# Recurrent attention with two mixtures of experts: the first expert's G spread in block order, with both spreadings ahead of the copies

## What is computed

```python
B, H, S, D = 4, 8, 768, 48            # attention; tokens = B*S = 3072, width = H*D = 384
for t in range(S):                    # state: (B, H, D, D)
    cur = einsum('bhd,bhe->bhde', u * k[t], v[t])
    y[t] = einsum('bhd,bhde->bhe', r[t], state + cur)
    state = w * state + einsum('bhd,bhe->bhde', k[t], v[t])
x = y as (3072, 384)
logits = x @ phi                      # 32 slots: 8 experts x 4
d, c = softmax(logits, 0), softmax(logits, 1)
slot_out[e] = relu((d.T @ x)[e] @ w1[e]) @ w2[e]
x = c @ slot_out                      # (3072, 384), rank 32
logits = x @ w_gate                   # 8 experts, top 1
e = argmax(logits, 1); g = softmax(logits, 1)[e]
out[n] = g[n] * (relu(x[n] @ w1b[e]) @ w2b[e])      # F = 1024 inner columns
```

## Time and profile before

| | |
|---|---|
| median of 3 runs | 275.95 us (275.84 to 276.87) |
| the profiled execution's own time | 276.53 us |
| its span, first to last instruction | 274.8 us |
| mean granted clock of TensorE, as a share of full | 0.975 |
| busy: PE, DVE, ACT, POOL | 95%, 56%, 32%, 11% |
| HBM traffic over the span | 200 GB/s |

### The profile page before, as it was taken

The page is one execution under the profiler, slowest core; times in us unless marked ns, Lnnn a source line. Parts: engine busy times, 40 slices in busy tenths (PEclk is TensorE's granted clock), DMA queues, the critical chain, the costliest instruction groups (busy, mean ns, idle before and its releaser), DMA issues.

```text
span 274.8 us, 10456 instructions
## 1 busy us (share of the span) xinstructions
PE 262.1 (95%) x4509; PEld 220.7 (80%) x4509; DVE 155.0 (56%) x322; ACT 89.3 (32%) x175; POOL 30.6 (11%) x45
## 2 busy tenths in 40 slices
PE   7979899999999998999999799999999999999996
PEld 6767687888787884433469599999999999999995
DVE  7957788888988874435030585353533522525323
ACT  1224445545545543031230453222222222222200
POOL 3312122222222215000000000000000000000000
PEclk9979999999999999999995979999999999999999
DMA  5955899999999999999507500030030200300303
GB/s 158 374 178 196 281 324 377 398 384 397 396 401 397 327 417 416 425 371 425 249 2 262 198 2 0 0 116 0 0 114 0 80 35 0 114 0 0 117 0 120
DMA packets 16260, 55.30 MB, mean 201 GB/s; under 512 B 1872, under 2 KB 5136, under 8 KB 15344
## 3 DMA queue, kind: packets, MB, share of 16 engines
q1 hardware_dynamic: 13152, 43.90, 42.7%
q10 hardware_dynamic: 3088, 11.14, 10.6%
HBM read 50.31 MB, written 4.72 MB: 200 GB/s over the span
## 4 chain that ended last, share of the span: by engine, by line
PE 91%; DVE 4%; issue 2%; ACT 1%; POOL 0%; DVEq 0%; POOLq 0%
PE ps L1207 12%; PE ps L1208 12%; PE ps L1206 12%; PE ps L939 8%; PE ps L962 6%; PE ps L977 6%; PE ps L986 5%; PE ps L951 5%; PE ps L1191 4%; PE ps L1077 4%; PE ps L1099 4%; PE ps L991 3%; PE ps L896 3%; PE ps L1046 2%; PE ps L1108 1%
## 5 line engine op out<-in xcount | busy, mean ns | idle before, releaser
L829 DVE SCALAR_TENSOR_TENSOR hl<-ps,hh 128x512 fp32r<-128x512 f32 x48 | 32.9, 690 | 58.5 <-ACT hh L571 58.5
L1207 PE MATMUL ps<-w2l,hh 128*128 128x384 f32 x192 | 65.2, 340 | 0.0
L1208 PE MATMUL ps<-w2h,hl 128*128 128x384 f32 x192 | 65.0, 338 | 0.0
L1206 PE MATMUL ps<-w2h,hh 128*128 128x384 f32 x192 | 64.9, 338 | 0.0
L571 ACT ACTIVATE hh<-ps 128x512 fp32r<-128x512 f32 x48 | 28.6, 598 | 75.6 <-PE ps L1191 75.6
L1207 PEld LDWEIGHTS ps<-w2l,hh 128*128 128x128 f32 x192 | 36.4, 190 | 1.6
L1206 PEld LDWEIGHTS ps<-w2h,hh 128*128 128x128 f32 x192 | 36.5, 190 | 0.7
L1208 PEld LDWEIGHTS ps<-w2h,hl 128*128 128x128 f32 x192 | 36.5, 190 | 0.0
L438 POOL TENSOR_TENSOR kt<-intk,kttab 128x384 f32<-128x384 f32 x24 | 24.2, 1008 | 71.1 <-DVE rkb L643 52.2
L643 DVE TENSOR_TENSOR rkb<-ind,tab 128x1024 f32<-128x1024 f32 x24 | 29.8, 1242 | 0.2 <-DMA ind<-dmaj 0.2
L939 PE MATMUL ps<-rkb 64*64 64x128 f32 x768 | 28.2, 279 | 0.0
(11 more groups left out here) (167 smaller groups left out, 304.0 us busy)
## 6 DMA issues: line engine op xcount, KB each, us to landing
ind<-dmaj SPq DMA_DIRECT2D x22, 512.0 KB, 7.8
wearly<-wa ACTq DMA_DIRECT2D x21, 512.0 KB, 7.2
intk<-tmaj SPq DMA_DIRECT2D x24, 384.0 KB, 6.8
wearly<-wa SPq DMA_DIRECT2D x4, 1536.0 KB, 10.4
out<-acc SPq DMA_DIRECT2D x5, 768.0 KB, 3.6
wlate<-wa SPq DMA_DIRECT2D x4, 768.0 KB, 8.8
wlate<-wa SPq DMA_DIRECT2D x2, 1536.0 KB, 11.3
wmid<-wa SPq DMA_DIRECT2D x1, 1536.0 KB, 8.6
```

Of the source, the lines that this page charges most:

```text
L829: v.scalar_tensor_tensor(out=hl[:, f % 4, :], in0=ps[:, f % 4, :], scalar=0.0, in1=hh[:, f % 4, :].bitcast(F32), op0=ALU.max, op1=ALU.subt ...
L1206: mm(o, a_h, w2h[:, f, :], start=(f == 0), stop=False)
L1207: mm(o, a_h, w2l[:, f, :], start=False, stop=False)
L1208: ins = mm(o, a_l, w2h[:, f, :], start=False, stop=(f == KF - 1))
```

## The change

Four things are edited. (1) G's columns: strip j now takes blocks j and j+4 (`w1cols`, a view of the same weights with two runs of 128 columns), so spreading 0 yields blocks 0 to 3 and spreading 1 blocks 4 to 7; `gstv` follows. (2) Both spreadings are issued back to back, then all copies: every copy of ScalarE waits for the third `gg_done` and every copy of VectorE for the fourth, so each of these engines copies both halves in a row. The first four `h1` are in block order; the first waits for ScalarE's first copy, the second for VectorE's first, the fourth for both second copies. (3) ScalarE makes `w2_high(0)` ahead of its copies instead of behind the first. (4) Products of ones: 3 new ones ahead of the wait for the last part of `cs`, 16 in place of 8 among the 24 gate products, none in place of 6 behind the gate, 2 new ones between the three parts of G, 1 new one behind the spreadings and 2 behind the four `h1`. The diff:

```diff
--- before.py
+++ after.py
@@ -157,7 +157,8 @@
                     piece[2 * e + 1].rearrange("p (f d) -> p f d", f=KF))
 
         w1raw = wraw[:, 0, :].rearrange("p (k f) -> p k f", k=KD)
-        gstv = gst[:, :].rearrange("p (j i n) -> p j i n", j=4, i=2)
+        w1cols = wraw[:, 0, :].rearrange("p (k i j n) -> p k j i n", k=KD, i=2, j=4)
+        gstv = gst[:, :].rearrange("p (i j n) -> p j i n", j=4, i=2)
         w2raw = wraw[:, 1, :].rearrange("p (f d) -> p f d", f=KF)
 
 
@@ -548,7 +549,7 @@
 
                 def g_copy(i):
 
-                    sc.wait_ge(gg_done, k * 4 + 2 * i + 1)
+                    sc.wait_ge(gg_done, k * 4 + 2 + 1)
                     a.activation(gstv[:, 0:2, i, :],
                                  ps[:, 4:6, i * P:(i + 1) * P], ACT.Copy).then_inc(gst_ready[2 * i], 1)
 
@@ -557,10 +558,9 @@
                     sc.wait_ge(w2b_in[first // 2], k * 16 + 16)
                     a.activation(w2h[:, first:end, :], w2raw[:, first:end, :], ACT.Copy).then_inc(w2h_done, 1)
 
-                def high(u, f, place=None):
-
+                def high(u, f):
                     n = k * NU + u
-                    sc.wait_ge(h_done, n * KF + (f if place is None else place) + 1)
+                    sc.wait_ge(h_done, n * KF + f + 1)
 
                     if f < 3:
                         sc.wait_ge(l2_done, n * (KF - 1) + f - 2 + L20)
@@ -572,12 +572,12 @@
 
                 sc.wait_ge(g_done, k + 1 + 1)
                 a.activation(gh[:, :], ps[:, 3, 0:F // 4], ACT.Copy).then_inc(gh_ready, 1)
+                w2_high(0)
                 g_copy(0)
-                w2_high(0)
+                g_copy(1)
                 high(0, 0)
-                g_copy(1)
                 w2_high(1)
-                high(0, 1, 2)
+                high(0, 1)
                 for p in range(2, len(W2P)):
                     w2_high(p)
                     high(0, 2 * p - 2)
@@ -813,7 +813,7 @@
 
                 def g_copy(i):
 
-                    dve.wait_ge(gg_done, k * 4 + 2 * i + 2)
+                    dve.wait_ge(gg_done, k * 4 + 4)
                     v.tensor_copy(gstv[:, 2:4, i, :],
                                   ps[:, 6:8, i * P:(i + 1) * P]).then_inc(gst_ready[2 * i + 1], 1)
 
@@ -1142,12 +1142,12 @@
             pe.wait_ge(gws_ready, 1)
             pe.wait_ge(cs_ready, 1)
             mm(ps[:, 4, 0:E], cs[:, 0:P], gw[:, :], start=True, stop=True).then_inc(gate0_done, 1)
+            warm(3, 6)
             pe.wait_ge(cs_ready, 6)
             for q in range(NT):
-                warm(q % 3 // 2, 6)
+                warm((q + 1) % 3 // 2 + q % 3 // 2, 6)
                 ins = mm(ps[:, 5, q * E:(q + 1) * E], cs[:, q * P:(q + 1) * P], gw[:, :], start=True, stop=True)
             ins.then_inc(gate_done, 1)
-            warm(6, 6)
 
 
             def expert(k, first):
@@ -1167,10 +1167,12 @@
                 pe.wait_ge(hl_done, k * J + 1)
                 pe.wait_ge(acc_done, k * NT + ACC0)
                 for q in range(KD):
+                    if first and q:
+                        warm(1, 0)
                     pe.wait_ge(w1b_in[q], k * 16 + 16)
                     for j in range(4):
                         ins = mm(ps[j * NS:(j + 1) * NS, 3, 0:W], sot[:, q, j * NS:(j + 1) * NS],
-                                 w1raw[:, q, j * W:(j + 1) * W], start=(q == 0), stop=(q == KD - 1),
+                                 w1cols[:, q, j, :, :], start=(q == 0), stop=(q == KD - 1),
                                  skip_group_check=True, tile_position=(0, j * NS))
                 ins.then_inc(g_done, 1)
                 if first:
@@ -1181,11 +1183,15 @@
                     warm(1, 0)
 
                 g_spread(0)
+                g_spread(1)
+                if first:
+                    warm(1, 2)
 
                 def h1(u, f, lead=False):
 
                     if lead:
-                        pe.wait_ge(gst_ready[f % 2 * 2], k + 1)
+                        if f < 2:
+                            pe.wait_ge(gst_ready[f], k + 1)
                     else:
                         pe.wait_ge(hl_done, (k * NU + u) * KF + f - 3 + 1)
                     mm(ps[:, f % 4, :], gst[:, f * P:(f + 1) * P],
@@ -1211,13 +1217,13 @@
                     if f < KF - 1:
                         ins.then_inc(l2_done, 1)
 
-                h1(0, 0, True)
-                h1(0, 2, True)
-                pe.wait_ge(gst_ready[1], k + 1)
-                g_spread(1)
-                pe.wait_ge(gst_ready[3], k + 1)
-                h1(0, 1, True)
-                h1(0, 3, True)
+                for f in range(4):
+                    if f == 3:
+                        pe.wait_ge(gst_ready[2], k + 1)
+                        pe.wait_ge(gst_ready[3], k + 1)
+                    h1(0, f, True)
+                if first:
+                    warm(2, 4)
                 with pe.Fori(0, NU - 1) as u:
                     for f in range(KF):
                         h2(u, f)
```

## The result

The changed kernel takes 273.44 us (median of 20 executions, 271.59 to 277.15), the kernel before 276.14 us on the same chip (20 executions, 272.57 to 279.26). The ratio is 0.9935, 95% interval [0.9911, 0.9958]: 1.8 us, 0.65%, less. That ratio leaves out executions more than 1.5% above the fastest of their kernel, eight of the twenty of the kernel before and one of the changed one; by the medians of all 20 and 20 it is 0.990, 2.7 us less. Either way it is faster, and by clearly less than the 4.2 us forecast (by the means of all, 276.12 to 273.59, it is 2.5 us). The profiled execution of the changed kernel, on the other hand, took 272.10 us where the sum had said 272.3.

What follows compares the result with a forecast made beforehand. TensorE was taken as the bound, with much of the edited stretch lost to ones, waits and half clock. Savings of 1.9 + 0.7 + 1.6 = 4.2 us gave a median of 271.7 us, own range 270.8 to 272.7, 8-in-10 range 270.6 to 274.7.

Steps and rivals of the forecast that it cites:

- it stood 0.58 above the median, so the median becomes 271.7: Whole kernel: the profiled 276.53 us becomes 272.3; carried over to the median of 275.95, this gives 271.7 us.
- Gate and G: Gate through G: denser ones keep full clock and the six ones go; spreading 0 at 153.1, 1.9 us sooner.
- and cost nothing: Within G: two thirds of G and two new ones (0.46) fit ahead of the last weights landing at 151.2.
- The wait for a DMA near 151.2: Sign of being right: G's last part waits for its weights near 151.2 us.
- Spreadings to the first `h2`: From spreading 0 to the first `h2`: copies behind both spreadings, first `h2` at 156.1, with 0.7 us saved here.
- First `h2`: First `h2` to the second: full clock through ones and four `h1` in a row, 2.32 in place of 3.88, 1.56 saved.
- What is late next: Behind the first `h2`: VectorE's fourth `split` ends by 163.6, ahead of the fifth `h2` at 165.4, covered by 1.8.
- All three: Rivals: full clock in only one place (0.17), ones not holding the clock (0.08), change only partly working (0.12).
- The slower rival: Gate: the ones do not hold the clock, the gate ends 3.9 us later than forecast, 277.3 us; chance 0.08.
- full clock in one of two places: Either the first `h2` stays slow or the gate goes slow for a while: 273.3 us; chance 0.17.
- 0.5 and 0.69: Upper side of the forecast's own range: 0.5 us for the read and the spreading, 0.69 for uncovered ones.

Runs made afterwards that it cites:

- after_thin_gate: Changed kernel with the gate's ones as before: 8 among the gate products, none ahead of the last wait, none behind the gate; ratio 1.0003 to the kernel before.
- look_before_1: Kernel before, unedited, one further profile; 18.98 us from L1144 to the second `h2`, 10.67 of it to spreading 0.
- order_only: Changed kernel with the products of ones put back as before, so only block order, spreadings and copies differ from the kernel before; ratio 1.0022 to it.
- gate_only: Kernel before with only the ones of the gate and G placed as in the changed kernel; old block order and copies; ratio 1.0009 to the kernel before.
- after_bare_lead: Changed kernel without the one product of ones behind the spreadings and the two behind the first four `h1`; ratio 0.9948 to the kernel before.
- r_after: Changed kernel run again without edit; ratio 0.9935 to the kernel before, mean 273.62 us.
- r_after2: Changed kernel run once more without edit, on another chip; ratio 0.9943 to the kernel before, mean 273.43 us.
- no_six: Kernel before without the six products of ones behind the gate, nothing else; ratio 1.0029 to the kernel before, median 277.40 us.
- r_before: Kernel before run again without edit; ratio 1.0017, mean 276.19 us, times from 273.44 to 279.56 us.
- look_before_2: Kernel before, unedited, a second further profile; 19.98 us from L1144 to the second `h2`, 13.90 of it to spreading 0.
- no_six_early: Kernel before without the six ones behind the gate and with w1b loaded sooner, always that of expert 0; ratio 1.0001 to the kernel before.

## Why the prediction was wrong, by its own steps

**The sum was right for the execution it was made from, and that execution was not the typical one.** The step that failed is the one from 276.53 - 4.2 to 275.95 - 4.2, "it stood 0.58 above the median, so the median becomes 271.7", together with pricing both edits at half clock: the terms of 1.9 (gate and G) and 1.6 (first `h2`) were taken as owed in every execution. The profiled execution had a clock of 0.975, that is (1 - 0.975) x 2 x 275 = 14 us at half clock (two falls in the edited stretch, and one from 15.6 that no edit touched). Over 104 executions the kernel before averaged 0.9856, 7.9 us; only 20 of them were at 0.975 or below. The changed kernel averages 0.9970, 1.65 us. So 6.3 us of half clock went away, not 14. Its price, from the mean of the 0.975 group against that at 1.00, is (277.83 - 273.28) / 13.8 = 0.33 us for each us at half clock: 2.1 us. Add the 0.5 us between the kernels at 1.00 (273.28 to 272.81) and the sum is 2.6, against 2.4 measured by means (275.93 to 273.56) and 2.9 by medians (276.10 to 273.24). This is a grouping of executions, not an edit; the edit that bears it out is after_thin_gate, whose clock of 0.983 is 7.7 us more at half clock than the changed kernel's: at 0.33 that is 2.5, less the 0.5 that its gate is shorter, and 1.9 was measured. How the gain splits between the terms of 1.9 and 1.6 over all executions stays open, since only the profiles show where the clock fell. I had three times of the kernel before, within 1.0 us, and took them for its scatter; it is 272 to 280.

**Gate and G, forecast 1.9.** Against its own profile 12.30 to 10.57, 1.7: right for that pair. Against the old gate at full clock (10.67 in look_before_1, 10.45 in order_only) nothing is left that can be told. I had the fact for this in hand, that w1b holds G until 151.2, and used it only for the kernel after. Used for the kernel before at full clock it says that six ones of 1.4 us end at about 149.3, ahead of the weights, and that nothing is gained.

In the changed kernel this part had a wrong sum as well. I let two thirds of G and the two new ones end ahead of 151.2 "and cost nothing", but 149.98 + 1.0 (two thirds of G's 1.50) + 0.46 is already 151.44. Each of those ones also took 0.42 us of TensorE's time between the parts of G, not 0.23. The chain that ended last in the first profile, and its line that loads w1b (issues, then the times to landing):

```profile
149.19 0.57 PE ps L1174 x8
149.76 0.42 PE ps L896 x2
150.18 0.57 PE ps L1174 x8
```

```profile
L382 SPq DMA_DIRECT2D wraw<-wb x3: 333/343/352, 144.4 to 145.5; - x3
DMA to landing us min/median/max: 3.8/4.5/5.3
```

The last third of w1b had landed at about 145.5 + 5.3 = 150.8, and G's last part began at 151.10, without a wait. The wait for a DMA near 151.2 that I had named as a sign of being right is in none of the three profiles of the changed kernel (gate_only and after_bare_lead, with the same gate, do wait there, 0.25 and 0.26 us). By this estimate the ones within G cost 0.3 us in the first profile, and 0.5 and 0.4 in r_after and r_after2 by their own loads. What they earn by the clock is not known, as they were not taken out alone.

**Spreadings to the first `h2`, forecast 0.7.** 3.74 to 3.15, 0.6: right, and in every profile with the clock up there. It is the one firm part, and about the 0.5 us between the kernels at 1.00. The second spreading took 0.27 (152.57 to 152.84) for which I had put 0.2. The read of the weights in two runs cost nothing: eight records of G are 0.64 long, as in look_before_1's last third and no_six's first, which read one run at full clock.

**First `h2`, forecast 1.6.** 3.88 to 2.44, 1.4 in the first pair; but r_before and look_before_2 have 2.33 and 2.34 without any edit. Here the slow case was in two of four profiles of before. I had credited the full clock here to the ones and the four `h1` in a row. The profiles say otherwise: of the eight with 8 ones in the gate (four of before, order_only, no_six, no_six_early, after_thin_gate) five have a first `h2` of 3.37 to 4.43 us, of the six with 12 or 16 ones in the gate none is above 2.44, and after_bare_lead is among these without any ones in the lead. So in these fourteen profiles the clock of the first `h2` goes with the denser gate ahead of it; by what is not shown. The last 0.1 of 2.44 against 2.34 lies in its first product, which starts behind a wait of 0.37 us for VectorE's `low`.

**What is late next.** Right: the fourth `split` reached nothing. Between the start of the first `h2` and 180 us TensorE's only wait is the 0.37 us for `low`, at that start.

**The rivals.** All three took the two falls of the kernel before as given and asked only whether the changed kernel would keep them. None asked how often the kernel before has them. The slower rival did not come: the clock held in the gate in all three profiles of the changed kernel, and 42 of its 44 executions were at 0.993 or above, which leaves room for one short fall at most in each of those. The 273.44 lies inside the range of 270.6 to 274.7, but for another reason than "full clock in one of two places". A slip in the range: 0.5 and 0.69 above 271.7 give 272.9, not 272.7; it changes nothing here. On the idle gaps that the Trainium skill (TensorE: Matmul & The Clock Gate, section "Why this matters for your kernels") names as the cause, the later profiles decide little. The first fall of the first profile of before still speaks against them as the only cause, since TensorE was busy for 1.89 of the 1.90 us ahead of it; in look_before_1 the clock fell at 154.7, 2.5 us behind an idle gap of 1.22 us and amid the waits for copies.

## What to carry to other kernels

Before pricing an edit by the clock, find out how often the clock is down there: the granted clock of each execution beside its time says whether the profiled one is typical, and three times are too few for it. A filler counts as work only if what it delays is not waiting for something else; here the load of w1b held G behind the six ones once the old gate ran at full clock. And a product that fills a wait can be worth more than its time by the clock (no_six gained nothing from removing 2.4 us of ones, and its mean clock fell from 0.985 to 0.975), so take it out alone before believing either.

## What the hardware showed that I had not expected

The same program at the same inputs took 272.0 to 280.4 us on one core, on each of three chips in turn (and once 357.19, at a clock of about 0.65), and its mean clock went from 0.963 to 1.00 in steps of about 0.006, one step being a fall of 3.4 us. Where the clock fell differed: at 15.6, 145.3 and 159.0 us in one profile of before, at 145.0 alone in the next, at 154.7, and at 30.1 and 146.1.

Ahead of the gate, executions also differ by waits that the profile puts to issue in the first passes of the attention loop. The changed kernel, waits of TensorE between 13 and 36 us in the first profile:

```profile
PE ps L951 <- issue: 1.7, 2, 1.4
PE ps L991 <- issue: 1.1, 1, 1.1
PE ps L977 <- issue: 1.0, 2, 0.7
```

and in r_after's:

```profile
PE ps L991 <- issue: 2.0, 1, 2.0
PE ps L951 <- issue: 1.7, 2, 1.4
PE ps L977 <- issue: 1.5, 2, 1.2
```

L1144 started at 142.00 in the one and at 144.84 in the other, with a fall of the clock at 30.8 us in the latter; from there on both took 16.16 us to the second `h2`. So what scatters in the changed kernel, in this pair, is all ahead of the edited stretch. What sets those waits was not tried.
